# Attention outputs formed by dimensions and sent through memory to the rows of the features

## The reference

```
# stage 1: delta rule attention, q, k, v: (4, 8, 768, 48), beta: (4, 8, 768)
k_n = k / (norm(k) + 1e-6);  state = 0                   # state: 48 x 48 per batch and head
for t in range(768):
    y[t]  = q[t] @ state
    state = state + beta[t] * outer(k_n[t], v[t] - k_n[t] @ state)
x = y as (3072 tokens, 384 features)                     # feature = head * 48 + dimension
# stage 2: x1 = relu(x @ w_in)**2 @ w_out                # 384 -> 2048 -> 384
# stage 3: g = x1 @ w_gate;  out = (g * sigmoid(g) * (x1 @ w_val)) @ w_out2   # 384 -> 1536 -> 384
```

## Time and profile before

| | before |
|---|---|
| time of the profiled execution | 1051.96 us |
| its span | 1050.2 us |
| median of three runs | 1053.46 us |
| PE busy | 990.0 us (94%), 10752 instructions |
| DVE / ACT / POOL busy | 408.2 / 302.9 / 207.8 us |
| X: transposes on PE | 72, 10.7 us busy |
| X: x_hi on ACT, x_lo on DVE | 24 each, 10.7 and 12.4 us |
| Y: evacuation on ACT | 46 copies of 128x192, 11.5 us |
| Y: instructions on PE | 704 with the state, 768 with qk |
| DMA | 74392 packets, 73.88 MB, 53168 of them under 512 B |

### The profile page before, as it was taken

How to read it: one execution, slowest core, us unless ns; L and a number is a source line. 1 busy time by engine, 2 the same in 40 slices (tenths; PEclk the granted TensorE clock), 3 DMA queues, 4 the chain that set the end, 5 groups by cost and what they waited for, 6 DMA issues and landing times.

```text
span 1050.2 us, 24211 instructions
## 1 busy us (share of the span) xinstructions
PE 990.0 (94%) x10752; PEld 821.9 (78%) x10752; DVE 408.2 (39%) x693; ACT 302.9 (29%) x599; POOL 207.8 (20%) x337
## 2 busy tenths in 40 slices
PE   2179999999999999999999999999999999999998
PEld 2178899778778878878888788888888888888886
DVE  3966644435434534543256521322312312312222
ACT  2225333333323333332345421221212211212211
POOL 1186481039307703920000000000000000000000
PEclk9999999999999999999999999999999999999999
DMA  7656423431441052130054010100100100100000
GB/s 230 190 158 190 141 74 87 131 92 52 123 134 62 31 147 86 51 107 23 2 175 156 1 61 1 49 12 1 61 1 1 61 1 1 61 1 0 31 1 31
DMA packets 74392, 73.88 MB, mean 70 GB/s; under 512 B 53168, under 2 KB 53296, under 8 KB 74288
## 3 DMA queue, kind: packets, MB, share of 16 engines
q1 hardware_dynamic: 68624, 64.99, 20.9%
q10 hardware_dynamic: 5664, 7.34, 2.2%
HBM read 56.59 MB, written 15.73 MB: 69 GB/s over the span
## 4 chain that ended last, share of the span: by engine, by line
PE 87%; POOL 4%; DVE 4%; DMA 2%; issue 1%; SPq 1%; ACT 0%; ACTq 0%; DVEq 0%; POOLq 0%
PE bank L887 86%; POOL prod L395 2%; POOL tinv L398 2%; DVE first_tinv L398 1%; DVE first_prod L395 1%; DMA tri_scratch<-gram 1%; SPq L414 1%; PE bank L1016 1%; DMA k_dim<-in_kt 0%; DMA first_tri<-tri_scratch 0%; DVE h_lo L853 0%; DMA tri<-tri_scratch 0%; DMA inv_scratch<-tinv 0%; POOL tri L389 0%; SPq L406 0%
## 5 line engine op out<-in xcount | busy, mean ns | idle before, releaser
L887 PE MATMUL bank<-x_hi,w_hi 128*128 128x512 f32 (+1 forms) x768 | 294.5, 383 | 1.2 <-DVE x_lo L828 1.2
L887 PE MATMUL bank<-x_lo,w_hi 128*128 128x512 f32 (+1 forms) x768 | 289.1, 376 | 0.0
L887 PE MATMUL bank<-x_hi,w_lo 128*128 128x512 f32 (+1 forms) x768 | 288.7, 376 | 0.0
L887 PE MATMUL bank<-h_hi,w_hi 128*128 128x512 f32 (+1 forms) x552 | 210.8, 382 | 4.8 <-DVE h_lo L853 4.8
L887 PE MATMUL bank<-h_lo,w_hi 128*128 128x512 f32 (+1 forms) x552 | 204.8, 371 | 0.0
L887 PE MATMUL bank<-h_hi,w_lo 128*128 128x512 f32 (+1 forms) x552 | 204.8, 371 | 0.0
L871 DVE TENSOR_TENSOR stage<-bank,stage 128x512 f32<-128x512 f32 x72 | 49.8, 692 | 318.5 <-ACT stage L741 318.5
L887 PEld LDWEIGHTS bank<-x_hi,w_hi 128*128 128x128 f32 x768 | 144.4, 188 | 29.5 <-DVE x_lo L828 1.6
L887 PEld LDWEIGHTS bank<-x_hi,w_lo 128*128 128x128 f32 x768 | 144.5, 188 | 26.6
L887 PEld LDWEIGHTS bank<-x_lo,w_hi 128*128 128x128 f32 x768 | 144.6, 188 | 24.7
L847 DVE TENSOR_TENSOR stage<-stage,bank 128x512 f32<-128x512 f32 (+1 forms) x112 | 68.4, 611 | 224.2 <-ACT stage L714 224.2
(11 more groups left out here) (84 smaller groups left out, 577.6 us busy)
## 6 DMA issues: line engine op xcount, KB each, us to landing
w_raw<-in_w SPq DMA_DIRECT2D x12, 576.0 KB, 3.8
k_dim<-in_kt SPq DMA_DIRECT2D x12, 512.0 KB, 4.7
q_dim<-in_qt SPq DMA_DIRECT2D x12, 512.0 KB, 3.8
k_prep<-in_kt SPq DMA_DIRECT2D x10, 512.0 KB, 3.9
x1s<-in_w ACTq DMA_DIRECT2D x12, 384.0 KB, 5.1
k_sq<-in_ky SPq DMA_DIRECT2D x12, 384.0 KB, 4.4
v_tok<-in_vy SPq DMA_DIRECT2D x12, 384.0 KB, 3.8
x_scratch<-x1s SPq DMA_DIRECT2D x18, 256.0 KB, 3.0
```

The source lines that it names most:

```text
L887: return pe.matmul(dst, lhsT, rhs, start=start, stop=stop, **kw)
```

## The change

From chunk 2 on (tile 1 on) Y forms its outputs by dimensions: the operands of its matmuls change places, so that 48 dimensions stand on the partitions and 64 tokens along the row. ACT copies them to `y_dim`, which has one buffer. SP stores `y_dim` to the DRAM tensor `y_dram` (two DMAs per chunk, 256 B pieces, `store_y`) and loads it back with the features on the partitions (`load_x`) into parts of `x1s`, columns 0 to 255 for the even and 512 to 767 for the odd chunk. The stage X of tiles 1 to 5 has nothing on TensorE and takes no bank. It comes in three parts (thirds of the features), one at slot 31 and two at slot 33. Each is an ACT copy and a DVE subtraction with both operands in SBUF. The first up of a unit waits for each third before its matmuls. Chunks 0 and 1 stay as they were. In SP's order `store_y` and `load_x` of a chunk stand ahead of `load_q` of the next, and `store_x1` goes by units.

```diff
+        def store_y(n):                                  # SP
+            for ready in y_ready:
+                sp.wait_ge(ready, 2 * (n + 1))
+            for ab in range(2):
+                sp.dma_start(y_dram[n].rearrange("(h d) (b x t) -> x d b h t", d=D, b=2, t=C)[ab],
+                             y_dim[ab * C:ab * C + D, :, :, :, :].rearrange("d b a r t -> d b (a r) t")
+                             ).then_inc(y_stored, 16)
+
+        def load_x(n):
+            t, s = divmod(n, 2)
+            if s == 0:
+                if t == 1:
+                    sp.wait_ge(x1_stored, 16 * KC)
+                else:
+                    sp.wait_ge(x1_stored, x1_kept(t - 2))
+            if t > 1:
+                sp.wait_ge(x_ready, features(t - 1, KC - 1))
+            sp.wait_ge(y_stored, 32 * (n - 1))
+            sp.dma_start(x1s[:, :, s * T:s * T + T // 2], y_dram[n].rearrange("(k p) t -> p k t", p=P)
+                         ).then_inc(x_loaded, 16)
...
             load_ky(5)                                   # SP's order, unit 1
 
+            store_x1(0)
+            store_y(2)
+            load_x(2)
             load_q(3)
             load_ktok(3)
             load_v(4)
+            store_y(3)
+            load_x(3)
             load_k(4)
...
                     store_both(2 * p + 1)                # SP's order, unit u = t from 2 on
+                store_y(2 * t)
+                load_x(2 * t)
                 load_q(n1)
                 if n1 < NCH - 1:
                     load_ktok(n1)
...
                     load_ky(2 * p + 1)
+                store_y(n1)
+                load_x(n1)
+                if p < NIT:
                     load_q(n2)
...
-                    for g in range(4):                   # plan(u)
-                        put(30 + g // 3, "X", t, g)
+                    for kc in range(KC):
+                        put(31 + 2 * (kc > 0), "X", t, kc)
...
+                    if name == "Y" and n > 2:            # ACT, before the evacuation
+                        act.wait_ge(y_stored, 32 * (n - 2))
...
+                elif name == "X" and n > 0:              # ACT
+                    kc = stage_[2]
+                    act.wait_ge(x_loaded, 32 * n)
+                    act.wait_ge(up_filled, NF1 * (n + 1))
+                    copy(x_hi[:, kc, :].rearrange("p (s t) -> p s t", s=2), x_raw(kc)).then_inc(x_hi_ready, 1)
...
+                elif name == "X" and n > 0:              # DVE
+                    kc = stage_[2]
+                    dve.wait_ge(x_hi_ready, features(n, kc))
+                    dve.tensor_tensor(x_lo[:, kc, :]..., x_raw(kc), x_hi[:, kc, :]..., ALU.subtract
+                                      ).then_inc(x_ready, 1)
...
                 if c > 0:                                # ACT and DVE, before the copies to x1s
-                    act.wait_ge(x1_stored, 16 * KC * c)
+                    act.wait_ge(x1_stored, x1_kept(c - 1))
+                if 0 < c < NIT - 1 or c0 > 0:
+                    act.wait_ge(x_ready, features(c + 1, KC - 1))
...
+                                    if n > 1:            # PE, q_state
+                                        at = (4 * bp + a) * C
+                                        mm(pair[r ^ flip][dims(ab), at:at + C], state[dims(r), m, :], q_dim[dims(r), m, :],
+                                           start=(flip == 0 and a == 0), stop=False, skip_group_check=True)
+                                        continue
...
+                                    if n > 1:            # PE, qk_u
+                                        at = (4 * bp + a) * C
+                                        done = mm(pair[bp ^ flip][dims(ab), at:at + C], u_tok[toks(bp), ab, 4 * r + a, :],
+                                                  qk[toks(bp), r, 2 * a + ab, :], start=False, stop=True,
+                                                  skip_group_check=True)
+                                        continue
...
-                pe.wait_ge(x_ready, 2 if u == 0 else 4 * (c + 1))
+                if c == 0:
+                    pe.wait_ge(x_ready, 2 * (u + 1))
...
                         for kc in range(KC):
+                            if c > 0 and f == 0:
+                                pe.wait_ge(x_ready, features(c, kc))
```

More of the change, by code:

```diff
@@ L82, in program @@
         u_tok = sb(att_mem, "u_tok", [P, 2, 8, D])
+        y_mem = ExitStack()
+        y_dim = sb(y_mem, "y_dim", [P, 2, 4, 2, C])
+        y_mem.close()
         y_tok = sb(att_mem, "y_tok", [P, 2, 2, 4, 2, D])
@@ L158, in program @@
         y_ready = [sem(f"y_ready{i}") for i in range(2)]
+        y_stored = sem("y_stored")
+        x_loaded = sem("x_loaded")
         ds_filled = sem("ds_filled")
@@ L276, in plan @@
                         put(25, "scale", p0)
-                    for g in range(4):
-                        put(30 + g // 3, "X", t, g)
+                    for kc in range(KC):
+                        put(31 + 2 * (kc > 0), "X", t, kc)
                 else:
@@ L304, in program @@
         for one in [one for u in range(NIT + 1) for slot in range(SLOTS) for one in PLAN[u].get(slot, [])]:
-            if one[0] in MATMULS:
+            if one[0] in MATMULS and (one[0] != "X" or one[1] == 0):
                 count = 1 if one[0] == "X" else 2
@@ L328, in emptied, with features, x1_kept, x_raw @@
                 return [(state_ready, 2 * (n + 1))]
-            return [(x_ready, 4 * n + stage_[2] + 1)]
+            return [(x_ready, features(n, stage_[2]))]
+        def features(c, part):
+            return (4 + KC * (c - 1) if c > 0 else 0) + part + 1
+        def x1_kept(c):
+            return 16 * KC * (c + 2)
+        def x_raw(kc):
+            return x1s[:, kc, :].rearrange("p (s t) -> p s t", t=T // 2)[:, 0:3:2, :]
         def dims(r):
@@ L371, in take_out @@
                 for bp in range(2):
-                    copy(y_tok[:, n % 2, bp, :, part ^ bp, :],
-                         bank[:, bp * 4 * D:(bp + 1) * 4 * D].rearrange("p (a d) -> p a d", d=D)
-                         ).then_inc(y_ready[part], 1)
+                    if n < 2:
+                        copy(y_tok[:, n, bp, :, part ^ bp, :],
+                             bank[:, bp * 4 * D:(bp + 1) * 4 * D].rearrange("p (a d) -> p a d", d=D)
+                             ).then_inc(y_ready[part], 1)
+                    else:
+                        copy(y_dim[:, bp, :, part ^ bp, :],
+                             bank[:, bp * 4 * C:(bp + 1) * 4 * C].rearrange("p (a t) -> p a t", t=C)
+                             ).then_inc(y_ready[part], 1)
         FILLED = {"G": g_filled, "U": u1_filled, "Z": z_filled, "Y": y_filled}
@@ L564, in _ @@
                     store_both(2 * p)
-                store_x1(u - 2)
+                store_x1(u - 1)
                 load_v(n1)
@@ L588, in load_x1 @@
             def load_x1(c):
[L589 removed]
+                sp.wait_ge(x1_stored, x1_kept(c))
                 if c > 0:
@@ L601, in _ @@
                 if f == 0:
-                    store_x1(NIT - 2)
+                    store_x1(NIT - 1)
                 if f == RING:
                     load_x1(0)
-            store_x1(NIT - 1)
+            store_x1(NIT)
             def store_out(c):
@@ L824, in run @@
                             dve.tensor_tensor(part, part, BANKS[stage_][bp][:, 0:8 * D], ALU.add).then_inc(state_ready, 1)
+                elif name == "X" and n > 0:
+                    kc = stage_[2]
+                    dve.wait_ge(x_hi_ready, features(n, kc))
+                    dve.tensor_tensor(x_lo[:, kc, :].rearrange("p (s t) -> p s t", s=2), x_raw(kc),
+                                      x_hi[:, kc, :].bitcast(f32).rearrange("p (s t) -> p s t", s=2), ALU.subtract
+                                      ).then_inc(x_ready, 1)
                 elif name == "X":
-                    dve.wait_ge(x_hi_ready, 4 * n + stage_[2] + 1)
+                    dve.wait_ge(x_hi_ready, stage_[2] + 1)
                     cols = slice(stage_[2] * P, (stage_[2] + 1) * P)
@@ L860, in _ @@
                 if c > 0:
-                    dve.wait_ge(x1_stored, 16 * KC * c)
+                    dve.wait_ge(x1_stored, x1_kept(c - 1))
+                if 0 < c < NIT - 1 or c0 > 0:
+                    dve.wait_ge(x_ready, features(c + 1, KC - 1))
                 for kc in (0, 2):
```

19 lines of the change are left out of this document (10 added, 9 removed).

## The result

| | before | after |
|---|---|---|
| median of four runs each, us | 1053.37 (1051.49 to 1053.81) | 1062.76 (1059.35 to 1064.13) |
| ratio | | 1.0084, 95% interval [1.0067, 1.0101] |
| span of the profiled execution, us | 1050.2 | 1062.4 |
| mean granted clock of TensorE | 0.999 | 0.994 |
| PE busy, us (instructions) | 990.0 (10752) | 986.7 (10692) |

The account below looks back on a forecast made before the run. From 67 us on, what TensorE issues plus its rare waits was taken as the time. Terms -7.0 + 0 + 2.2 + 0.2 = -4.6 gave 1047.4, plus 0.9 for a typical run 1048.3 us; range 1043.6 to 1053.0.

Parts of the forecast that it names:

- Step 1: At five unit ends, removing the 12 transposes per tile (tiles 1 to 5) gains 1.39 us each, 7.0 us in all.
- Step 2: Y's matmuls with operands exchanged, 48 stationary and 64 moving columns: cost 0, with 4.6 us kept for the range.
- DS's price: Stage DS's 13.4 ns per matmul (48 and 48 columns); for Y it would give 0.46 us per chunk, 4.6 in all.
- Rival B: Y also gets the matmul price of stage DS, gaining 4.6 us more: 1044.7 us; chance 0.20.
- Step 3: ACT's copies of Y take at most 1.33 us instead of 1.00, the x split is hidden: cost 0.
- Step 4: On SP, q's load behind Y's store and reload: path 9.4 us, stall 2.2 (1.5 to 4.3) in unit 1, full units 0.
- x: Microseconds by which the path from Y filled to QK is longer than 9.4; from 2.0 the kernel is slower.
- rival C: q is late for QK in every unit, behind the store's landing; at 3 us more path, 1058 us; chance 0.20.
- Step 5: U asks for the inverses earlier at three unit boundaries: cost 0.2 us, up to 4.2 if U had no spare.
- D: The inverse chain takes back the transposes' gain, 4.2 us lost instead of 0.2: 1052.3 us, no change; chance 0.15.

Follow-up runs that it names:

- no_transposes_late: The kernel before without the transposes of tiles 1 to 5, and the split's pieces moved from slots 30 and 31 to 31 and 33: 1046.78 us, 0.9934.
- no_transposes: The kernel before with the transposes of X left out for tiles 1 to 5, nothing else changed: 1052.08 us, 0.9986.
- long_pieces: The changed kernel with Y stored in 4 KB pieces, one per partition, instead of 256 B pieces: 1058.61 us, 1.0043.
- x_psum: The changed kernel with x_lo's first operand read from PSUM instead of SBUF, and each unit's first up waiting for all thirds: 1056.33 us, 1.0020.
- both_early: The changed kernel with q and the triangles loaded ahead of Y's store, and the lane step at slot 14 instead of 16: 1045.28 us, 0.9927.
- q_first: The changed kernel with SP issuing the load of q for the odd chunk (chunk 3 in unit 1) ahead of Y's store: 1053.79 us, 1.0001.
- kept_busy: The changed kernel with unread matmuls added before the unit 1 wait for q (18) and three waits for inverses (9 each): 1058.47 us, 1.0045.

## Why the prediction was wrong, step by step

**Step 1 (transposes), right in size.** 6.42 us at the unit's end against 6.4, and -6.5 by no_transposes_late against -7.0. The working treated the split's new slots as a side matter ("can't delay it"); without them the unit ends gained nothing (no_transposes).

**Step 2 (Y), right.** 0.08 us a chunk gained, where DS's price would have given 0.46. Rival B is out.

**Step 3 (evacuations), half right.** ScalarE's copies took 1.21 us against 1.00 and cost nothing by themselves. The split's thirds were put down as "hidden", which holds for TensorE; that their operands now lie in SBUF, and what this does to GpSimd, was not asked.

**Step 4 (SP's queue), the step that failed first.** The mechanism and the place were right, the landing was not. It was taken from 64 KB stores at 3.2; from the first issue to the reload's it gave 3.8 (with the issues), and was 5.46 in unit 1 and 4.3 to 5.8 at the other chunks. With q's own landing 4.3 instead of 3.8, the path was 143.72 - 132.26 = 11.5 us from Y filled to QK, where 9.4 stood. That is x = 2.06, just past the point 2.0 from which rival C was slower: q waits of 4.4 in unit 1 and 3.5 in the full units (C at that x: 4.3 and 3.0). The rows at hand were of another size and count of pieces: each DMA here has 768 pieces of 256 B, three times the bytes of the rows used. That the pieces are what delays it, long_pieces shows. With its late landing of 5.3 the step's own terms add up to 11.5 (it said 11.4, and 8.6 where its short row gives 8.8), and that is what came. The case stood in rival C, but the range, which ended at 1053.0, left it out.

**Step 5 (inverses), failed by more.** 0.2 was said, 6.9 came, beyond the 4.2 of its bound. At the first boundary the spare of 1.4 was there and the unit's shorter end used it up, as worked out. On top came 1.3 of longer solve, of which x_psum shows 1.0, and 0.95 of later landing of the inverse's store (2.62 us from its issue to the first load's before, 3.57 after): 2.25 together, and the wait is 2.37. At the other two the same terms give 3.2 and 1.7, and the waits are 2.50 and 2.26: right in sum, not one by one. The bound had assumed that solve and loads stay as they are. Why that store lands later isn't settled: single boundaries at 3.5 to 4.5 us occur in both_early, and in no_transposes and no_transposes_late, which have none of the new DMAs, but the changed kernel and q_first have all three above 3.2.

**What no step held: the clock.** TensorE's granted clock went to 1.2 GHz after three of the four waits of over 2 us. 4.8 us by the trace and 4.3 by kept_busy, of 19.6 us of losses in all, paid behind the waits.

C and D did not exclude each other. I gave them chances as alternatives (0.20 and 0.15), and both came true together, with the clock's share on top: -7.8 (steps 1 and 2) + 7.9 + 6.9 + 4.8 = +11.8. D alone is q_first, and it came out at 1.0001.

## What to carry to other kernels

Removing work from the bounding engine makes every deadline behind it come earlier. List each chain beside it (load, solve, store and reload) with its spare, and price a change against the smallest spares together, not one by one. When a wait enters a queue, ask who stands behind it, and put the loads that are due soonest ahead of it: here such moves turned +0.8% into -0.7%. When an operand moves from PSUM to SBUF, look at what GpSimd does in that moment.

## What the runs showed of the hardware

- A subtraction of 128x512 on VectorE with both operands in SBUF takes 0.68 us alone and up to 1.09 (median of 15 pieces: 1.03) with GpSimd working beside it; with one operand in PSUM it stays at 0.68. GpSimd's solve took 45.77 us with the first and 44.77 with the second. Of two such operations that meet, the one that started first kept its time (`h_lo` 0.69 from 250.60 on in the changed kernel, GpSimd 0.64 from 249.49 on before the change) and the other took 1.15 and 1.14.
- A store of 192 KB landed in 3.5 us (median of twenty, 3.2 to 5.1) in 256 B pieces and in 2.6 (2.4 to 4.1) in 4 KB pieces, and its issue took 0.64 us against 0.38.
- After idle stretches of 4.41, 2.50 and 2.26 us TensorE's granted clock went down to 1.2 GHz and cost 1.7, 1.5 and 1.6 us; after one of 2.37 it didn't. Over the traces of all kernels, from unit 1 on, the matmuls behind 11 of 15 waits of over 2 us were slow; one of 2.05 was among them and one of 2.46 wasn't, so the length of the wait alone doesn't tell. Unread matmuls in the gap kept the clock at 2.4 GHz.
